# Merging two key blocks with a predicated copy in PSUM, and moving three transposes in the schedule

## The reference

```python
# attention: 4 sink keys and a window of 128 keys back
scores = q @ k.T / sqrt(64)
keep = (key < 4) | ((0 <= query - key) & (query - key < 128))
a = softmax(where(keep, scores, -1e9))            # denominator + 1e-9
x = a @ v
# MLP, weights [512, 2048] and [2048, 512]
h = x @ w_in
x2 = (h - tanh(h)) @ w_out
# routing to one of 8 experts, weights [512, 1024] and [1024, 512] each
e = argmax(x2 @ w_gate + modality_bias[modality_id])
out = gate_weight * (relu(x2 @ w1[e]) @ w2[e])
```

## Time and profile before

| | us |
|---|---|
| median of 3 runs | 1071.74 |
| lowest, highest | 1071.53, 1072.14 |
| the profiled execution, as timed | 1070.08 |
| its span in the trace | 1068.1 |
| startup and tiles alone (to the first `mlp_in`) | 84.2 |
| windows 0 to 7 | about 690 |
| experts' stage | about 294 |

### The profile page before, as it was taken

The page is one execution under the profiler, slowest core; times in us unless marked ns, Lnnn a source line. Parts: engine busy times, 40 slices in busy tenths (PEclk is TensorE's granted clock), DMA queues, the critical chain, the costliest instruction groups (busy, mean ns, idle before and its releaser), DMA issues.

```text
span 1068.1 us, 23850 instructions
## 1 busy us (share of the span) xinstructions
PE 989.9 (93%) x7968; PEld 605.0 (57%) x7968; DVE 650.4 (61%) x2272; ACT 581.4 (54%) x1329; POOL 327.3 (31%) x462
## 2 busy tenths in 40 slices
PE   2748999999999999999999999999899999899996
PEld 1524444555554555555455556555487777677774
DVE  6665767667768767777866775646765334633331
ACT  4766786666667765766666675536422224522221
POOL 5766675112116211213511210101032232232322
PEclk9958999999999999999999999999999999999999
DMA  8710001201100320100210010041024211111111
GB/s 315 256 36 19 18 19 66 79 19 35 48 18 19 64 79 19 49 18 19 37 48 19 19 48 1 2 159 59 1 51 174 75 49 54 40 41 49 49 47 40
DMA packets 24375, 60.30 MB, mean 56 GB/s; under 512 B 9504, under 2 KB 9760, under 8 KB 22752
## 3 DMA queue, kind: packets, MB, share of 16 engines
q1 hardware_dynamic: 15392, 45.77, 13.2%
q0 software_dynamic: 5728, 13.43, 4.0%
q10 hardware_dynamic: 3168, 0.02, 0.1%
HBM read 45.35 MB, written 14.12 MB: 56 GB/s over the span
## 4 chain that ended last, share of the span: by engine, by line
PE 73%; DVE 12%; ACT 6%; issue 5%; POOL 1%; DVEq 1%; DMA 1%; ACTq 0%; SPq 0%; POOLq 0%
PE h_ps L751 19%; PE acc L807 18%; PE h_ps L1907 5%; PE s_ps L1856 5%; PE pt_ps L1856 5%; PE acc L1907 5%; PE pt_ps L639 4%; PE s_ps L569 3%; PE x_out L706 3%; ACT probs L587 2%; PE s_ps L858 1%; DVE qk_top L401 1%; PE pt_ps L662 1%; DVE pt_lo L648 1%; PE x_out L1833 1%
## 5 line engine op out<-in xcount | busy, mean ns | idle before, releaser
L807 PE MATMUL acc<-w_out_all,g_hi 128*128 128x512 f16 x768 | 228.4, 379 | 0.0
L751 PE MATMUL h_ps<-xt_hi,w_in_all 128*128 128x384 f16 x960 | 196.8, 328 | 4.2 <-DVE g_raw L772 3.0
L807 PE MATMUL acc<-w_out_all,g_lo 128*128 128x512 f16 x384 | 146.0, 380 | 3.3 <-DVE g_lo L792 2.7
L751 PEld LDWEIGHTS h_ps<-xt_hi,w_in_all 128*128 128x128 f16 x960 | 91.3, 100 | 62.3 <-issue 7.4
L807 PEld LDWEIGHTS acc<-w_out_all,g_hi 128*128 128x128 f16 x768 | 75.1, 98 | 77.7
L763 ACT ACTIVATE g_raw<-h_ps,batch_scale 128x384 f32<-128x384 f32 x120 | 69.5, 579 | 89.2 <-PE h_ps L751 85.3
L792 DVE SCALAR_TENSOR_TENSOR g_lo<-g_raw,batch_scale,g_hi 128x384 f16<-128x384 f32 x128 | 84.6, 661 | 44.4 <-ACT g_hi L782 44.4
L782 ACT ACTIVATE g_hi<-g_raw,batch_scale 128x384 f16<-128x384 f32 x128 | 77.9, 608 | 55.4 <-DVE g_raw L772 54.0
L101 POOL TENSOR_TENSOR tick<-tick 1x1 f32<-1x1 f32 x83 | 15.6, 188 | 293.4 <-ACT y L1923 116.2
L580 DVE CUSTOM_DVE_ANT_0 probs<-s_ps,mask 128x260 f32<-128x260 f32 (+1 forms) x192 | 70.0, 402 | 49.7 <-issue 43.9
L751 PE MATMUL h_ps<-xt_lo,w_in_all 128*128 128x384 f16 x480 | 98.3, 328 | 0.0
(11 more groups left out here) (315 smaller groups left out, 2098.2 us busy)
## 6 DMA issues: line engine op xcount, KB each, us to landing
qk_raw<-in_qk SPq DMA_DIRECT2D x31, 454.0 KB, 3.4
raw<-in_w SPq DMA_DIRECT2D x16, 512.0 KB, 8.1
v_raw<-in_v SPq DMA_DIRECT2D x4, 1536.0 KB, 7.0
x_tokens<-x SPq DMA_DIRECT2D x24, 256.0 KB, 2.5
w_in_all<-in_w_in SPq DMA_DIRECT2D x4, 1024.0 KB, 9.6
w_out_all<-in_w_out SPq DMA_DIRECT2D x4, 1024.0 KB, 9.0
x_tokens<-g_raw SPq DMA_DIRECT2D x1, 1024.0 KB, 12.7
vs_raw<-in_v SPq DMA_DIRECT2D x24, 4.0 KB
```

The lines of the kernel that those rows point to most:

```text
L751: mm = eng.matmul(h_of(m, f), w16[0][:, f, x * DM + k * P:x * DM + (k + 1) * P], r[:, par, k, :], start=(i == 0), stop=(i == 3 * KD - 1))
L807: mm = eng.matmul(acc[t][:, :], l[f % 2][:, t * P:(t + 1) * P], w16[1][:, f, x * DM:(x + 1) * DM], start=(f == 0 and i == 0), stop=(f == N ...
```

## The change

The block before and the tile's own block never both hold a visible key in one column: query `i` sees key `j` of its own block where `j <= i`, and key `j` of the block before where `j > i`. The changed kernel merges them: DVE copies the scores of the block before over the hidden half of the own block, in PSUM (`copy_predicated`, with a constant triangle `past` as predicate), and the columns that follow are 132 in place of 260.

- `score_pair` on DVE: one predicated copy of 2x128 columns for both heads (2x132 with a constant for a first tile; a further one of 2x4 columns for the tiles of `a` even and `t` 1), then, after a wait for it, one `tensor_reduce` over 2x132 columns, in place of the two custom instructions. The scale 1/8 is put into the scale of the queries and keys (`SCALE_BITS`).
- ACT takes the exponential from PSUM, 132 columns for each head. The scores' banks are so read until the exponentials are done: PE's next scores, and the routing's use of `s_ps0`, wait for `exped` where they waited for `shifted`.
- `normalise`: one pair of DVE instructions for both heads; ACT products of 132 columns.
- `transpose_probs`: two transposes in place of four; the split is 256 columns in place of 512 and goes to `merged`. POOL then parts it with `affine_select` into the two blocks that `weigh_values` reads, each a triangle with zeros in the rest: two instructions of 4x128 columns, one for a first tile. PE's `weigh_values` waits for this (`parted`).
- The low halves of `w_in` move from POOL (two instructions) to DVE (one), half a step or a slot later than before. Those of `w_out` stay on POOL.
- In `mlp_out` the sinks' transposes stand after the third output tile, not after the second.

The core of the diff:

```diff
@@ constants (POOL): the mask becomes a triangle of ones, and a constant
-                eng.memset(mask[:], 0.0).then_inc(q["masked"], 1)
+                eng.memset(later[:], 0.0).then_inc(q["masked"], 1)
+                eng.memset(never[:], NEG).then_inc(q["masked"], 1)
@@ weight_split
-            if E == "pool":
+            if E == "dve" and i == 0:
+                eng.wait_ge(q["w_hi0"], f + 1)
+                eng.scalar_tensor_tensor(lo, raw, w_scale[:, 0, 0:1], hi, ALU.mult, ALU.subtract).then_inc(q["w_lo0"], 1)
+            if E == "pool" and i == 1:
@@ score_pair
-                claim_scores(eng, (q["shifted"], 2 * r + 1))
-                need(eng, q["shifted"], 2 * r)
+                claim_scores(eng, (q["exped"], 2 * r + 2))
+                need(eng, q["exped"], 2 * r)
...
-                need(eng, q["normal"], 2 * (r - RING + 1))
-                m = mask[:, t if a % 2 == 0 else 2, cols]
-                eng.memset(tick[0:1, 4:5], 0.0)
-                for j in range(2):
-                    eng.tensor_tensor_reduce(out=probs[:, r % RING, j, cols], in0=s_banks[j][:, cols], in1=m, scale=-SCALE,
-                                             scalar=3.0e38, op0=ALU.add, op1=ALU.min,
-                                             accum_out=neg_max[:, r % RING, j:j + 1]).then_inc(q["shifted"], 1)
+                if is_first(r):
+                    step(eng.copy_predicated(s_both[:, :, P:KW], past.unsqueeze(1).to_broadcast([P, 2, KB]),
+                                             never[:].unsqueeze(1).to_broadcast([P, 2, KB])))
+                else:
+                    if joins(r + 1) - joins(r) == 2:
+                        step(eng.copy_predicated(s_both[:, :, P:KB], past[:, SINK:2 * SINK].unsqueeze(1).to_broadcast([P, 2, SINK]),
+                                                 never[:].unsqueeze(1).to_broadcast([P, 2, SINK])))
+                    step(eng.copy_predicated(s_both[:, :, KB:KW], past[:, SINK:KB].unsqueeze(1).to_broadcast([P, 2, P]),
+                                             s_both[:, :, 0:P]))
+                eng.tensor_reduce(neg_max[:, r % RING, :], s_both[:, :, P:KW], AX.X, ALU.max, negate=True)\
+                   .then_inc(q["shifted"], 1)
             if E == "act":
+                eng.wait_ge(q["shifted"], r + 1)
+                need(eng, q["normal"], 2 * (r - RING + 1))
                 for j in range(2):
-                    x = probs[:, r % RING, j, cols]
-                    eng.wait_ge(q["shifted"], 2 * r + j + 1)
-                    eng.activation(x, x, ACT.Exp, bias=neg_max[:, r % RING, j:j + 1], scale=-1.0,
-                                   accum_out=row_sum[:, r % RING, j:j + 1]).then_inc(q["exped"], 1)
+                    eng.activation(probs[:, r % RING, j, :], s_banks[j][:, P:KW], ACT.Exp, bias=neg_max[:, r % RING, j:j + 1],
+                                   scale=1.0, accum_out=row_sum[:, r % RING, j, 0:1]).then_inc(q["exped"], 1)
@@ transpose_probs
-                    for b in range(first, 2):
-                        mm = eng.transpose(out[:, j, b - first, :], normed[:, 2 * t + j, b * KB:b * KB + P], ident[:])
+                    mm = eng.transpose(out[:, j, :], normed[:, 2 * t + j, SINK:KB], ident[:])
...
+            if E == "pool":
+                at = pt[:, 0:24, :].rearrange("p (x t b) c -> p x t b c", t=TPC, b=2)[:, :, t]
+                both = merged[:, r % RING].rearrange("p x j c -> p (x j) c")
+                eng.wait_ge(q["pt_lo_done"], m + 1)
+                need(eng, q["pv_done"], pv_count(TPC * (g - 1) + (1, 2, 2)[t]))
+                eng.affine_select(out=at[:, :, 1, :], in_=both, pattern=[[0, 4], [1, P]], compare_op=ALU.is_ge, fill=0.0,
+                                  base=0, channel_multiplier=-1).then_inc(q["parted"], 1)
+                if not is_first(r):
+                    eng.affine_select(out=at[:, :, 0, :], in_=both, pattern=[[0, 4], [-1, P]], compare_op=ALU.is_gt, fill=0.0,
+                                      base=0, channel_multiplier=1).then_inc(q["parted"], 1)
@@ weigh_values
-                eng.wait_ge(q["pt_lo_done"], turned(r) + (2 if last else 1))
+                eng.wait_ge(q["parted"], parts(r))
+                if last:
+                    eng.wait_ge(q["pt_lo_done"], turned(r) + 2)
@@ mlp_out
-                    if t == 1 and between:
+                    if t == 2 and between:
@@ alone; window has the same with "and even" and ago(2)
+                if E == "pool":
+                    stage(transpose_probs, E, eng, r - 1)
```

121 lines of the change are left out of this document (63 added, 58 removed).

## The result

| | before | changed |
|---|---|---|
| median of 18 runs each, us | 1073.42 (1070.43 to 1074.96) | 1069.86 (1065.84 to 1071.54) |
| profiled execution, us (span) | 1070.08 (1068.1) | 1065.96 (1064.4) |

The ratio is 0.9966, 95% interval 0.9956 to 0.9975: faster, by 3.6 us, where 18 were forecast, and outside the range of 1043 to 1065. Both profiled executions lie at the quick end of their kernel's runs, so the traces can be set side by side.

What follows compares the result with a forecast made beforehand. PE bounds the windows, chains through four engines the first 84.2 us. Windows 1 to 6 give 13.0 + 3.0, window 0 2, the first part 0: 18.0 us off, 1053.7 us, range 1043 to 1065.

Steps and rivals of the forecast that it cites:

- PE's work: Windows 1 to 6: 59 tiles each save 0.22 us of transposes, 13.0 us off PE.
- PE's wait for the sinks: Slot 23 of windows 1 to 5: shorter wait for the sinks' low half, 0.6 us each, 3.0 us off.
- what is late next?: Window 1, after the sinks' wait: `g_raw` must come 0.8 us earlier; DVE saves 0.26 on low half, about 0.3 on reciprocals.
- Scores on DVE: Copy and reduction take 0.89 us, 0.11 more than before; covered by the 0.50 us before `g_raw` is needed, cost nothing.
- Rival D: A slow predicated copy makes `g_raw` late in every tile's slot; at 1.4 us a copy, 1077 us; chance 0.08.
- Sharing with DVE: POOL's selects can delay DVE, but follow where it turns to `g_raw`, reading PSUM, and `g_lo` has slack: no charge.
- The selects in window 0: POOL's unbroken run grows 2 us, weighings of slots 24 and 26 wait; window 0 gains 2 us, ends -4 and 5.
- The held bank: Score bank held until the exponentials: about 1.2 us once before `L324` in window 0, about 1.3 in the first part.
- Everything behind is about 1.3 later: First part: PE's second scores, at 9.67, also wait for ACT, shifting everything behind by about 1.3 us.
- DVE's new `w_in` work: First part: ten low halves of 744 ns fall between DVE's key scales on the chain, +3 us.
- POOL's relief: First part: POOL loses ten `w_in` slices, gains 22 selects; its first run +1 us, `k_lo` -2.
- C: Rival: first part grows as POOL waits for DVE's low half and DVE carries weights; 6 us off, 1065; chance 0.16.

Runs made afterwards that it cites:

- experiment 7: The changed kernel with the sinks' transposes back behind the second output tile, timed: 1065.13 us against 1071.98 for the kernel before, ratio 0.994.
- experiments 5 and 6: Sinks' transposes at the old place in the changed kernel, at the new in the kernel before; new place in windows 1 to 6: +3.5 and +1.7 us.
- Experiment 1: The changed kernel with each POOL select cut from 128 columns of a head to 8: windows 1 to 6 513.45 us against 515.2.
- experiment 4: The changed kernel with the low halves of `w_in` back on POOL: first part 91.2 us (+3.5), windows 1 to 6 515.9.
- experiment 2: The kernel before with score banks held until the exponentials: first part 87.5 us (+3.3), window 0 99.3 (+2.9), windows 1 to 6 unchanged.
- experiment 9: The changed kernel with DVE's next-batch steps ahead of the sinks' low half and sinks' transposes behind the second output tile: windows 1 to 6 508.7 us.
- experiment 12: The changed kernel with a second pair of score banks in the first part and next-batch steps ahead of the sinks' low half: 1057.94 us, ratio 0.9863.

## Why the prediction was wrong

Step by step, in its own order:

- **PE's work, -13.0 in windows 1 to 6:** right. Busy time fell from 514.4 to 502.7 us with the dip, and to 500.9 in the changed kernel of experiment 7, which had no dip and the same transposes of `normed`.
- **PE's wait for the sinks, -3.0:** the wait of slot 23 fell from 0.97 to 0.47 us, near enough. The step "what is late next?" failed. It named `g_raw` and covered its 0.8 us with 0.26 saved on the low half and 0.3 on reciprocals. No reciprocal stands there ahead of `g_raw` in the trace of the kernel before, where DVE has `L619`, `L648`, `L923`, `L924` and `L772` in a row. The 0.26 came (0.67 to 0.40 for the low half), but `L944` beside the select took back 0.44, and PE's wait moved over whole: 0.79 us behind it. And the step looked forward to PE alone. What it left out is what stands behind the moved step on the other engines. Slot 15's row maximum and slot 7's maxima stand behind the sinks' low half on DVE, which starts 0.64 us later. That is +1.3 us in each of windows 2 and 4. Measured alone, the move is +1.7 in windows 1 to 6.
- **Scores on DVE, 0:** right in price and in effect. Rival D (a copy of 1.07 us or more) is out at 0.43.
- **Sharing with DVE, "No charge":** wrong. It looked at `g_raw` (PSUM, never held) and `g_lo` and not at the routing and gate operations, which stand between the low half and `g_raw` in some slots, although the trace of the kernel before has `L924` at that very point (the line under experiments 5 and 6). Experiment 1 prices it at some 3 us. The other case that it names, the low halves of `w_in`, is small: three of 16 took 0.1 to 0.3 us longer than their median, and experiment 4 shows no cost. Nor did it see that the merged reciprocal, which it counts as a saving, would itself be held up (`L613`).
- **The selects in window 0, 2 us of gain there:** the waits for POOL's select came in the two slots named, 24 and 26, and in 28 (0.64, 0.66, 1.10 us at 157, 165 and 172), 2.4 us by experiment 1, and `L323` waits 1.09 where 1.2 stood. The wait for `g_raw` grew from 1.8 to 3.1 us, unforeseen. Net +0.4, within the ends of -4 and 5.
- **The held bank:** the step that failed in the first part. It was priced once at 1.3 us, at the second tile, and at one place of window 0. But PE waits for the exponentials in eight tiles of the first part, 9.8 us, and the hold alone makes that part 3.3 us longer (experiment 2). "Everything behind is about 1.3 later" took a cost per tile for a cost at the start.
- **DVE's new `w_in` work, +3, with POOL's relief -2 and +1:** reversed. The move to DVE is worth -3.5 (experiment 4). The wait for POOL's `k_lo`, 12.6 us in the earlier trace rows, is 10.7 with the move and 14.5 without, so POOL's relief counted and DVE's load did not show.
- **Clock:** a dip of 3.4 us in window 2 added 1.5. That is not in the sum, and not in every kernel run; the profiled execution of the kernel before has none in its windows. The timed runs differ here, too: the 18 of the changed kernel have a mean granted clock of 0.971 to 0.978, the lower ones mostly the longer, and nine later ones of the kernel before 0.976 to 0.981. What part of the missing time that is, no run separates.

In sum: 0 became +3.5, -2 became +0.4, and -16 became -7.5. For the last the waits tell what came in place of -3.0: those for the sinks and `g_raw` together went from 6.2 to 7.2 us (to 3.5 with the short selects of experiment 1, so the forecast would nearly have held there but for the selects), those for the row maximum and ahead of scores from 2.3 to 3.9, those for `normed` from 0 to 1.2, and the clock added 1.5. That is 5.3 where -3.0 was forecast. The nearest rival was C, 6 us off, and its cause was another one: not DVE's `w_in` work, but the bank. That C's number lies near is luck.

Open is what makes the clock stay at half for 3 to 5 or for 8 to 9 us into window 0. Experiment 2, experiment 9 and experiment 12 had the long form, the others the short one.

## What to carry to other kernels

When a step moves by 0.6 us on one engine, follow its chain to the other engines and list what is queued behind its last link there: what empties a shared bank must not stand behind something that waits. Before counting a gain at a wait, look at how soon the next instruction of the same releaser is needed. Work moved to POOL is paid for by DVE's tiny operations on SBUF, each of which can take as long as the POOL instruction beside it, so place it where DVE reads PSUM; merging two of one column into one of two columns can expose them to it. A buffer held longer cost nothing where long work of the same engine lay between two uses, and 3.3 us over 14 tiles where it did not; two buffers taken by turns gave most of that back.

## What the runs showed of the hardware

- A predicated copy of 256 float32 columns within PSUM under an SBUF mask takes 429 ns on DVE, 1.7 ns a column; with a broadcast scalar as source 490 for 264 columns and 226 for 8.
- A select of 512 float16 columns on POOL takes 0.63 us (the median of 96), and one of 32 columns 0.23.
- DVE operations of 3 or 24 columns took 0.17 to 0.19 us alone, 0.61 to 0.62 beside a select and 1.01 beside POOL's two-input operation of 1.15. `g_lo` (384 columns, 0.62 us) took up to 1.59 us, at 335.15, beside `L494` and `L512`. `g_raw`, with one input from PSUM, took 0.60 to 0.62 in all 128 cases.
- The same DVE operation took 133 to 155 ns on one column in 192 cases and 150 to 581 on two columns in 96, and the 44 of these that took over 200 all started while a POOL instruction ran and ended with it.
- A stretch at the lower clock level in the windows lasted 3.4 us each time and cost 1.4 to 1.6; at the start of window 0 it lasted 3 to 5 or 8 to 9 us, and the difference cost about 2.
